# Splitting the last network's weights: loads on GpSimd's queue, other places in the order, and output tiles transposed inside the sum buffer

## The reference

```python
# attention, 8 heads of 64, with 32 packed queries p
p_packed = softmax(scale * p @ k.T) @ v
x = softmax(scale * q @ p_packed.T) @ p_packed          # then (8, 576, 512)
# first network
xk = mu_k * x + (1 - mu_k) * x_prev;  xr = mu_r * x + (1 - mu_r) * x_prev
x = sigmoid(xr @ w_r) * (relu(xk @ w_k) ** 2 @ w_v)
# last network: tokens mixed at rank 32, then 512 -> 2048 -> 512
u = x + (x.T @ U @ V).T
out = u + relu(u @ w_ch1) @ w_ch2
```

## Time and profile before

| | us |
|---|---|
| median of 3 runs | 1508.77 (1506.27 to 1509.91) |
| the profiled execution | 1511.3 |
| its span, first to last instruction | 1508.9 |
| its mean granted clock of TensorE | 0.962 |
| TensorE busy | 1342.3 (89%) |
| VectorE, ScalarE, GpSimd busy | 976.6, 679.5, 170.9 |

### The profile page before, as it was taken

How to read it: one execution, slowest core, us unless ns; L and a number is a source line. 1 busy time by engine, 2 the same in 40 slices (tenths; PEclk the granted TensorE clock), 3 DMA queues, 4 the chain that set the end, 5 groups by cost and what they waited for, 6 DMA issues and landing times.

```text
span 1508.9 us, 21258 instructions
## 1 busy us (share of the span) xinstructions
PE 1342.3 (89%) x7592; PEld 1135.2 (75%) x7592; DVE 976.6 (65%) x1609; ACT 679.5 (45%) x1200; POOL 170.9 (11%) x214
## 2 busy tenths in 40 slices
PE   2379999999999997769879999999999997999997
PEld 1268777788888886657658777877888787989896
DVE  2667667667676755644565586748775585567766
ACT  1445464454545544534343454435443443454443
POOL 2700000000000034412310120002000110010000
PEclk9699999999999998989999999999999998999998
DMA  7744153232412067772896669765796568877986
GB/s 147 174 80 87 58 97 74 71 72 59 83 55 58 15 194 239 247 237 86 266 289 182 183 176 233 229 189 165 209 252 190 179 190 219 270 225 217 279 249 169
DMA packets 386792, 252.49 MB, mean 167 GB/s; under 512 B 249280, under 2 KB 302560, under 8 KB 386688
## 3 DMA queue, kind: packets, MB, share of 16 engines
q1 hardware_dynamic: 378720, 243.97, 58.4%
q0 software_dynamic: 1632, 5.40, 1.1%
q10 hardware_dynamic: 6336, 1.77, 0.5%
HBM read 201.25 MB, written 49.81 MB: 166 GB/s over the span
## 4 chain that ended last, share of the span: by engine, by line
PE 63%; DVE 11%; DMA 8%; SPq 8%; issue 4%; ACT 3%; POOL 2%; DVEq 0%; ACTq 0%; POOLq 0%
PE bank L1031 20%; PE bank L1113 18%; PE bank L773 9%; PE bank L787 7%; PE bank L752 3%; SPq L1234 3%; DMA piece_raw<-in_moe_w_ch 3%; DMA w_ring<-w_parts 2%; DVE mixed L725 2%; DVE hid_parts L1137 1%; DMA w_parts<-late_out 1%; SPq L1408 1%; PE bank L926 1%; DVE acc L1156 1%; PE bank L856 1%
## 5 line engine op out<-in xcount | busy, mean ns | idle before, releaser
L1031 PE MATMUL bank<-u_parts,w_ring 128*128 128x512 f32 (+1 forms) x1680 | 368.2, 377 | 25.2 <-DVE hid_raw L1072 9.9
L1113 PE MATMUL bank<-hid_parts,w_ring 128*128 128x512 f32 (+1 forms) x1680 | 361.1, 371 | 12.9 <-DVE hid_parts L1137 4.3
L1031 PEld LDWEIGHTS bank<-u_parts,w_ring 128*128 128x128 f32 x1680 | 312.2, 192 | 71.3 <-issue 28.9
L1113 PEld LDWEIGHTS bank<-hid_parts,w_ring 128*128 128x128 f32 x1680 | 302.8, 188 | 69.9 <-issue 25.3
L1131 ACT ACTIVATE hid_parts<-hid_raw 128x512 fp32r<-128x512 f32 (+1 forms) x280 | 164.5, 588 | 156.2 <-PE bank L1113 154.7
L1137 DVE TENSOR_TENSOR hid_parts<-hid_raw,hid_parts 128x512 fp32r<-128x512 f32 (+1 forms) x280 | 184.3, 662 | 59.7 <-ACT hid_parts L1131 54.6
L773 PE MATMUL bank<-xk_hi,wk_hi 128*128 128x384 f32 x384 | 132.8, 346 | 13.1 <-DVE xk_lo L744 8.5
L773 PE MATMUL bank<-xk_lo,wk_hi 128*128 128x384 f32 x384 | 130.3, 339 | 0.0
L773 PE MATMUL bank<-xk_hi,wk_lo 128*128 128x384 f32 x384 | 130.3, 339 | 0.0
L787 PE MATMUL bank<-wv_hi,k_hi 128*128 128x512 f32 x288 | 117.5, 408 | 2.8 <-DVE k_lo L823 2.8
L787 PE MATMUL bank<-wv_hi,k_lo 128*128 128x512 f32 x288 | 115.9, 402 | 0.0
(11 more groups left out here) (144 smaller groups left out, 1817.6 us busy)
## 6 DMA issues: line engine op xcount, KB each, us to landing
w_ring<-w_parts SPq DMA_DIRECT2D x560, 256.0 KB, 3.5
w_parts<-piece_out SPq DMA_DIRECT2D x24, 896.0 KB, 4.8
x_scratch<-x SPq DMA_DIRECT2D x36, 256.0 KB, 2.0
kq_parts<-in_k SPq DMA_DIRECT2D x120, 72.0 KB, 2.5
kq_parts<-in_q SPq DMA_DIRECT2D x112, 72.0 KB, 2.2
v_rows<-in_v SPq DMA_DIRECT2D x56, 128.0 KB
w_parts<-late_out SPq DMA_DIRECT2D x8, 896.0 KB, 6.7
out_dram<-out_rows SPq DMA_DIRECT2D x96, 64.0 KB, 2.9
```

What stands on the lines that cost most here:

```text
L1031: last = nc.tensor.matmul(to, wring[:, e % RW, ct, a, :], uc[:, pos, b, ct, 0:w], start=(pos in FRESH and ct == 0 and a == 0 and b == 0), ...
L1113: last = nc.tensor.matmul(role(st, j, BANK_OF[pos])[:, 0:w], wring[:, e % RW, j, a, :], hid[:, no % RH, b, 0:w], start=(pos in FRESH and i ...
```

## The change

- The loads of the pieces are issued by GpSimd instead of SP (`pool_pieces`). It issues the first `slots - 1` pieces' loads at once, and from then on, before the sums of piece n, it waits until piece n-1 is split and issues the loads of piece n + slots - 1. Early pieces have three slots, late ones two.
- 20 pieces are early instead of 24, and 12 late instead of 8. Piece n is split in slot 4 + 3n//2 and stored 2 slots later. The pieces' order changes from all of w1, then all of w2, to w1 and w2 of group 0, then w1 and w2 of group 1 (`piece_no`); before group 1's first ring load of a w1 part, SP waits for those late pieces.
- The late places are now six in stage 1 of the first pair (mostly 4 entries apart) and six in stage 2, at entries 3, 7, ..., 23.
- The second half's transposes move from (2,1), (2,4), (3,1), (3,4) to (2,5), (3,1), (3,3), (3,5) (`U_SPOTS`: unit, position). The loads keep their rule.
- An output tile k > 0 is transposed into the place of tile k-1 in the sum buffer and waits for the turn before it alone; only tile 0 goes to `out_rows`, of which one is left. The turns stand at position 3 of each unit of stage 1 and at entries 5, 11, 17 and 23 of stage 2. ScalarE waits for the output transfers before it fills a sum buffer again.
- The weight ring has 11 slots instead of 10; its last first load waits for two more groups of the first stage.

```diff
@@ -69,9 +69,9 @@
 NG, NU = 2, 4
 NPROD = 7
 PIECES = 2 * 2 * NG * NU
-LATE = PIECES // 4
+LATE = 12
 SLOTS_P = 3
-RW, RH = 10, 3
+RW, RH = 11, 3
 MIX_AT = (9, 10, 12, 14)
 WEIGHTS_AFTER = {"scores2": 1, "sm1": 3, "norm1": 2}
...
     plan = {}
-    for i in range(PIECES - LATE):
-        at = 3 * i // 2
-        plan.setdefault(at, []).append(("ws_load", i))
-        plan.setdefault(at + 2, []).append(("ws_split", i))
-        plan.setdefault(at + 3, []).append(("ws_store", i))
+    for n in range(PIECES - LATE):
+        at = 4 + 3 * n // 2
+        plan.setdefault(at, []).append(("ws_split", n))
+        plan.setdefault(at + 2, []).append(("ws_store", n))
     return plan
...
 LAST_SUM = {"11": "Y", "22": "X", "12": "Y", "21": "X"}
-LATE_SPOTS = [(0, i, pos) for i in range(1, NU) for pos in (1, 3, 5)] + [(1, 0, 2), (1, 0, 4)]
+LATE_SPOTS = [(0, 1, 1), (0, 1, 5), (0, 2, 2), (0, 2, 6), (0, 3, 1), (0, 3, 5)] + [(1, 0, e) for e in range(3, 27, 4)]
+
+
+U_SPOTS = [(0, 1), (0, 4), (1, 1), (1, 4), (2, 5), (3, 1), (3, 3), (3, 5)]
+TURN_AT = (5, 11, 17, 23)
 def late_pieces(spot):
     at = LATE_SPOTS.index(spot)
-    items = []
-    for kind, after in (("ws_split", 2), ("ws_store", 3), ("ws_load", 0)):
-        if 0 <= at - after < LATE:
-            items.append((kind, PIECES - LATE + at - after))
+    items = [("ws_split", PIECES - LATE + at)]
+    if at > 0:
+        items.append(("ws_store", PIECES - LATE + at - 1))
     return items
...
                 items += {0: [("ea", g, i)], 1: [("ez", g, i)], 2: [("eb", g, i)], 3: [("c11", g, i)],
                           4: [("relu", g, i, 0), ("c22", g, i)], 5: [("relu", g, i, 1), ("c12", g, i)],
                           6: [("relu", g, i, 2), ("c21", g, i)]}[pos]
-                if pos in (2, 3) and turns:
+                if g == 0 and pos == 3 and turns:
                     items += turns.pop(0)
                 if p == 0 and g == 0 and (0, i, pos) in LATE_SPOTS:
                     items += late_pieces((0, i, pos))
                 if g == 0 and i == 1 and pos == 0 and p < NB - 1:
                     items.append(("x_load", p + 1, 0))
-                if g == 1 and p < NB - 1 and pos in (1, 4):
-                    n = 2 * i + pos // 4
+                if g == 1 and p < NB - 1 and (i, pos) in U_SPOTS:
+                    n = U_SPOTS.index((i, pos))
                     items.append(("u", p + 1, n))
                     if n == 3:
                         items.append(("x_load", p + 1, 1))
...
             items.append(("m2", g, pos, i))
             if p == 0 and g == 0 and (1, 0, e) in LATE_SPOTS:
                 items += late_pieces((1, 0, e))
+            if p == 0 and g == 0 and e == NPROD * NU - 1:
+                items.append(("ws_store", PIECES - 1))
+            if g == 0 and e in TURN_AT and turns:
+                items += turns.pop(0)
             if e < 2:
                 items += [("t", g, NU - 1, 2 * e), ("t", g, NU - 1, 2 * e + 1)]
             if e + RH < NPROD * NU:
...
     with ExitStack() as early:
         piece_out += [sb(f"late_out{i}", [P, NPROD, 2, P], F32R, early) for i in range(2)]
     acc.append(sb("acc1", [P, CT, 2, CB]))
-    turned = [sb(f"out_rows{i}", [P, CB]) for i in range(2)]
+    turned = sb("out_rows", [P, CB])
     flat = lambda t: t[:, :, :].rearrange("p b n -> p (b n)")
...
         w = PAIRS_B[p][1]
         act.wait_ge(u_ps, 2 * CT * p + n + 1)
         if p > 1:
-            act.wait_ge(turn_ok, len(TILES) * (p - 1))
+            act.wait_ge(out_done[1], 64 * (len(TILES) - 1) * (p - 1))
         elif p == 1:
             for i in range(2):
                 act.wait_ge(piece_stored[SLOTS_P + i], 16 * LATE // 2)
...
         out_, j = TILES[k]
         no = len(TILES) * p + k
         dve.wait_ge(sum_ok, sum_no(p, NG - 1, SUM_AT[(out_, LAST_SUM[out_], j)]) + 1)
-        if no < 2:
+        if no == 0:
             dve.wait_ge(g_out, 16 * (B + 1))
+        elif k == 0:
+            dve.wait_ge(out_done[0], 64 * p)
         else:
-            dve.wait_ge(out_done[no % 2], 64 * (no // 2))
+            dve.wait_ge(turn_ok, no)
         nt, half = sum_place(out_, j)
-        nc.vector.transpose(turned[no % 2][:, 0:w].rearrange("p (m d) -> p m d", d=32),
+        nc.vector.transpose(turn_place(p, k).rearrange("p (m d) -> p m d", d=32),
                             acc[p % 2][:, nt, half, 0:w].rearrange("p (m d) -> p m d", d=32)).then_inc(turn_ok, 1)
+
+    def turn_place(p, k):
+
+
+        w = PAIRS_B[p][1]
+        if k == 0:
+            return turned[:, 0:w]
+        nt, half = sum_place(*TILES[k - 1])
+        return acc[p % 2][:, nt, half, 0:w]
+
+    def piece_no(n):
+
+
+        g, rest = divmod(n, 4 * NU)
+        product, rest = divmod(rest, 2 * NU)
+        return product, g, rest // 2, rest % 2
     def piece_slot(n):
...
         return (n % SLOTS_P, n // SLOTS_P) if n < early else (SLOTS_P + (n - early) % 2, (n - early) // 2)
     def piece_loads(n):
-        return 2 if n < 2 * NG * NU else 3
+        return 3 if piece_no(n)[0] else 2
+
+    def load_piece(pool, n):
+
+        slot, _ = piece_slot(n)
+        product, g, i, half = piece_no(n)
+        r = piece_raw[slot]
+        fa, fb = (2 * NU * g + i) * P, (2 * NU * g + NU + i) * P
+        if product == 0:
+            rows = w1.rearrange("(k c p) f -> p c k f", k=2, c=2, p=P)[:, half, :, :]
+            pool.dma_start(r[:, 1:5:3, :], rows[:, :, fa:fa + P]).then_inc(piece_in[slot], 16)
+            pool.dma_start(r[:, 0:8:7, :], rows[:, :, fb:fb + P]).then_inc(piece_in[slot], 16)
+        else:
+            cols = lambda f: w2[f:f + P, :].rearrange("p (k j n) -> p j k n", k=2, j=2)[:, half, :, :]
+            pool.dma_start(r[:, 1, :], cols(fa)[:, 0, :]).then_inc(piece_in[slot], 16)
+            pool.dma_start(r[:, 0, :], cols(fa)[:, 1, :]).then_inc(piece_in[slot], 16)
+            pool.dma_start(r[:, 4:8:3, :], cols(fb)).then_inc(piece_in[slot], 16)
     def pool_piece(pool, n):
         slot, turn = piece_slot(n)
...
         nc.gpsimd.tensor_tensor(r[:, 3, :], r[:, 2, :], r[:, 1, :], ALU.subtract).then_inc(piece_sum, 1)
         pool.wait_ge(piece_sum, 4 * n + 3)
         nc.gpsimd.tensor_tensor(r[:, 6, :], r[:, 4, :], r[:, 3, :], ALU.subtract).then_inc(piece_sum, 1)
+
+    def pool_pieces(pool, first, end, slots):
+        for n in range(first, first + slots - 1):
+            load_piece(pool, n)
+        for n in range(first, end):
+            if n + slots - 1 < end:
+                if n > first:
+                    pool.wait_ge(piece_lo, n)
+                load_piece(pool, n + slots - 1)
+            pool_piece(pool, n)
+
+    def pieces_stored(eng):
+
+        for i in range(SLOTS_P):
+            eng.wait_ge(piece_stored[i], 16 * len(range(i, PIECES - LATE, SLOTS_P)))
     def act_piece(act, n):
         slot, turn = piece_slot(n)
...
                 for i in range(CT, KQ):
                     load_z(sp, 0, i)
-        def load_piece(n):
...
         def store_piece(n):
             slot, _ = piece_slot(n)
-            unit_, half = divmod(n % (2 * NG * NU), 2)
-            g, i = divmod(unit_, NU)
+            product, g, i, half = piece_no(n)
             sp.wait_ge(piece_lo, n + 1)
-            if n < 2 * NG * NU:
-                to = w1_dram[unit_, :, :, half, :]
+            if product == 0:
+                to = w1_dram[NU * g + i, :, :, half, :]
             else:
                 to = w2_dram[g, :, :, i, half, :].rearrange("a p n -> p a n")
             sp.dma_start(to, piece_out[slot][:, :, :, :].bitcast(F32).rearrange("p a h n -> p a (h n)")
...
             if rest < NPROD * NU:
                 i, pos = divmod(rest, NPROD)
                 part = w1_dram[NU * g + i, :, pos, :, :]
+                if p == 0 and g == 1 and rest == 0:
+                    for n in range(PIECES - LATE, 6 * NU):
+                        slot, turn = piece_slot(n)
+                        sp.wait_ge(piece_stored[slot], 16 * (turn + 1))
             else:
                 pos, i = divmod(rest - NPROD * NU, NU)
                 part = w2_dram[g, pos, :, i, :, :]
...
                 sp.wait_ge(att.x_dve, 2 * B)
                 sp.wait_ge(scaled_prev, 4 * NCH)
                 sp.wait_ge(mix_ok, 4 * NCH)
-                for i in range(SLOTS_P):
-                    sp.wait_ge(piece_stored[i], 16 * ((PIECES - LATE) // SLOTS_P))
+                pieces_stored(sp)
                 for i in range(4):
                     sp.dma_start(v_stage[i * NP:(i + 1) * NP, :], vv).then_inc(v_in, 16)
                 load_x2(0, 0)
...
             elif item[0] == "b_ring":
                 sp.wait_ge(moe_ps, MOE_GROUPS * (NCH - 1) + NFA)
                 for e in range(RW):
+                    if e == RW - 1:
+                        sp.wait_ge(moe_ps, MOE_GROUPS * (NCH - 1) + KR)
                     load_ring(e)
-            elif item[0] == "ws_load":
-                if item[1] == 0:
-                    sp.wait_ge(att.x_act, 2 * B)
```

(24 more changed lines are left out.)

17 lines of the change are left out of this document (removed).

## The result

The changed kernel takes 1483.71 us (median of 4 runs, 1482.97 to 1486.93) against 1509.34 (1506.27 to 1512.24): ratio 0.9835, 95% interval 0.981 to 0.9859. Its profiled execution has a span of 1480.9 us where the old one had 1508.9.

A forecast was written before the change was run, and what follows sets the result against it. TensorE, busy 89% of the span, was taken as the bound, with only its idle time and slow clock winnable. Early pieces 6.5, late pieces 4, transposes 10.9 and outputs 12 sum to 33 us: 1476, range 1455 to 1499.

The forecast's parts named there:

- The loop of an early piece: Early stretch: GpSimd's issues, sums, split and hand-overs form one chain, 5.98 us, or 6.32 with a w2 load.
- What is left behind the last piece: Last early split to last stage: 50.3 us before, less 13.8, plus 10; last stage at 703, a gain of 6.5.
- The new one has 10 us more of groups: Behind the last early piece, now at slot 32 instead of 36, TensorE has 10 us more groups before the transposes.
- the last store lands by about 664: End of the early stretch: last store landed by 664, x2 tiles some 673, when TensorE arrives; the 11.3 us wait goes.
- The late pieces: First pair's late stretch, 12 pieces for 8: GpSimd's loops take 67.4 us against 59 of TensorE; gain 4 us.
- Transposes: Four pairs' stops before the fifth transpose all go when it moves 4 entries later: 10.9 us, bounds 9 to 12.
- Outputs: VectorE's waits for output transfers and the fourth pair's losses: two thirds of 18.5 us gained, 12; bounds 4 and 18.5.
- the ring has an eleventh slot: Weight ring in the last stage: given as one reason within the 12 us output term, without its own size.
- The change does nothing for the pieces, 1487: Rival on the pieces: ScalarE waits as long, both piece terms zero, 1487; inside the forecast's range, no chance of its own.
- Sums meet VectorE each time: Rival: GpSimd's sums always meet VectorE's backlog, 4.1 us instead of 2.3 a loop, 49 us more, 1525; chance 0.15.
- The rule quoted for it: VectorE instructions with two SBUF inputs contend with GpSimd's SBUF reads; second blocks; alone it would make the change slower.
- Loop short: Rival: GpSimd's sums meet no VectorE instruction, four in 1.8 us, half a us less in 27 loops, 1462; chance 0.17.

The follow-up runs named there:

- e7: e4 with each late store issued 2 entries behind its split instead of at the next split: 1451.78 us, ratio 0.9616.
- e5: e4 with the late pieces' sums, too, ahead of GpSimd's wait and loads, with two buffers: 1469.11 us, ratio 0.973.
- e1: The kernel before with only the new places of the x2 transposes' second half: 1496.23 us, ratio 0.9876.
- e2: The kernel before with only the output tiles turned inside the sum buffer and their new places, ring of 10 slots: 1498.84 us, ratio 0.9894.
- e2b: e2 with the eleventh ring slot added: 1501.24 us, ratio 0.990 to the kernel before.
- e13: The changed kernel with the old pieces (SP's loads, 24 early, 8 late), loads ahead of stores inside SP's slots: 1465.97 us, ratio 0.9693.
- e4: The changed kernel with GpSimd's early sums of a piece ahead of its wait and the next loads: 1454.29 us, ratio 0.9641.

## Why the prediction was right in time and where not

The forecast was 1476 and a range of 1455 to 1499; the time is 1483.7. Of the sum's four terms the two for the pieces were wrong and the two small parts right or too low: 10.5 us forecast and none measured for the pieces, 22.9 forecast and 29.6 measured for the rest. That the second error made up for more than half of the first is luck.

- **The loop of an early piece: right.** Forecast 5.98 and 6.32 us and 3 us over all, 107 for 17 loops; measured 105.0. The issues took 0.72 and 0.54 to 0.55 where 0.74 and 0.54 were taken from the earlier trace rows; the sums took 2.23 on average, 1.85 where they met nothing, instead of 2.30; one hand-over, VectorE to GpSimd's next issue, took 0.3 us and those to ScalarE and VectorE 0.03, where 0.15 stood for all four. The last piece was split at 654.0, forecast 656.5.
- **What is left behind the last piece: the step that failed.** "The new one has 10 us more of groups" was 17: it counts the four slots by which the last piece moved, and takes TensorE to be as far ahead of the splits as before. It was not. TensorE stood 10.55 us before 648.53 with a small product behind the queue of splits, and at the last split, in slot 32, still had the end of a v group (slot 33) and all eight k groups, 21.1 us. In the old kernel it had 3.7 left, slots 40 and 41, at the split of slot 36. Then "the last store lands by about 664" was 666.4, because SP held two stores behind the chunk's end, and TensorE stood 1.7 us for what SP issued next; and the faster clock gave 1.8 us of the 2.5. Together 56.3 us instead of 46.5, which is more than the gain of 6.5.
- **The late pieces: mis-sized.** 11 intervals took 79.0 us, not 71.4. Landings of GpSimd's loads were no trouble (5.3 us for 128 KB against a loop of 7.2; GpSimd waited 3.2 us for them in all). What I left out is shown only in part: the stores account for 4.9 us of ScalarE's waits, and e7, with its stores issued sooner, shortened group 0 by 1.1. What holds group 0 at 94 to 103 us in every version but e5 stays open; in the changed kernel nearly all of TensorE's waits there are ended by VectorE.
- **Transposes: right in cause, too small.** The stops go as forecast, the stretches give 15.0, in the whole change and in e1 alone, instead of 10.9. Only the idle time of the stops was counted. The other 4.1 us are busy time, 3.6 of it in the two stretches in which the granted clock fell behind the stop; for the fourth pair's stage 1 the prediction had counted the slow clock, here it did not.
- **Outputs: right, with a borrowed part.** 14.6 and 12 forecast, but part of the 14.6 comes with the transposes too, as e1 shows; by e2 and e2b 8.8 of the fourth pair's 10.5 us come from the turns, and the ring gives nothing over all, so "the ring has an eleventh slot" was an empty part of that term.
- **Rivals.** "The change does nothing for the pieces, 1487" is what happened to the pieces. "Sums meet VectorE each time" did not happen: the medians of the four sums are 0.46 to 0.47 us, and 20 of the 80 took more than 0.6 us, up to 1.19. The rule quoted for it (Trainium skill, "SBUF — State Buffer", Who interferes with whom) agrees with the trace for these: each of the 20 lies beside a VectorE instruction with two inputs. But just behind a split GpSimd mostly met none. "Loop short" had that three times in four, not each time, and the loop stayed at 6.18.
- **What no step of it said:** that the wait in GpSimd's loop stood ahead of work that does not need it. I wrote down the order (wait, issue, then sum) and priced it, but did not ask what the loop would be in the other order; it is worth 28 us of the stretch, more than the 25.6 us of the whole change.

## What to carry to other kernels

When loads move to another engine's queue, write down the loop that results: wait, issue, compute, and what the wait really guards. Work that needs no part of the wait belongs ahead of it; whether that helps is a matter of buffers, as three gave 28 us here and two lost 13. And count what the critical engine still has to do behind the last item of a stretch, not only when that item ends: four pieces fewer ended 5 us earlier and left 17 us more of groups behind them. Where a stop is taken away, look at the granted clock behind it too: two of the four stops, of 2.7 and 2.3 us, cost 1.8 us more each by it.

## What the runs showed of the hardware

GpSimd's issues took the same time whether VectorE was at work beside them or not, 710 to 765 ns for 128 KB; two rows of the changed kernel's view of `piece_raw` (ns min/median/max). The early loads landed about as fast from its queue as from SP's, 4.1 us for 128 KB against 4.3, though at a lower DMA share (0.63 against 0.78); the late ones took 5.3 against 4.7:

```profile
L1211 POOL DMA_DIRECT2D piece_raw<-in_moe_w_ch x12: 720/720/765, 523.7 to 641.5; - x12
...
L1217 POOL DMA_DIRECT2D piece_raw<-in_moe_w_ch x8: 710/710/712, 574.3 to 618.5; - x8
```

```profile
piece_raw<-in_moe_w_ch POOLq DMA_DIRECT2D x32, 128.0 KB, 4.1
...
late_raw<-in_moe_w_ch POOLq DMA_DIRECT2D x16, 128.0 KB, 5.3
```

The Trainium skill, "DMA: Bandwidth & Descriptors", Issuing engines are not separate DMA queues, says that issuing from several engines only saves the sequencer's time; the trace agrees, and e13 shows that the order of SP's list, not its issue time, was what the old kernel paid for. In e4, 45 of GpSimd's 80 sums took more than 0.6 us, up to 1.31, each beside a VectorE instruction with two inputs, and the loop was the shorter one all the same. I had not expected the unchanged part of the program to vary: the last pair starts between 528.2 and 533.5 us in fourteen profiled executions, which is more than several of the differences above.
